# Two expert layers in one program block: the second layer's setup lines up behind the first's last block

## The reference, cut to what matters

```python
# x: 4 sequences x 5056 tokens x 256; N = 20224 tokens, D = 256, E = 8 experts, F = 1024
h[t] = f[t] * h[t-1] + (1 - f[t]) * x[t]          # scan, f from f_logit and lower_bound
# layer 1: every expert takes exactly N/8 tokens, by rank over all (token, expert) logits
y[tokens of e] = relu(h[tokens of e] @ w1[e]) @ w2[e]
# layer 2: every token goes to its best expert, times that expert's softmax weight
e*, g = argmax, softmax of y @ w_gate2
out[t] = g[t] * (relu(y[t] @ w1b[e*]) @ w2b[e*])
```

## Time and profile before

| | us |
|---|---|
| three runs | 2419.19, 2417.88, 2418.66 (median 2418.66) |
| the profiled execution, its own time | 2422.26 |
| its span, from the first to the last instruction | 2420.5 |
| PE busy in the span | 2268.7 (94%) |
| mean granted clock of PE | 0.973 of full |
| last matmul of the first layer's last block, end | 1380.8 |
| first transpose of the second layer, start | 1411.8 |

### The profile page before, as it was taken

How to read it: one execution, slowest core, us unless ns; L and a number is a source line. 1 busy time by engine, 2 the same in 40 slices (tenths; PEclk the granted TensorE clock), 3 DMA queues, 4 the chain that set the end, 5 groups by cost and what they waited for, 6 DMA issues and landing times. The chain is left out here.

```text
span 2420.5 us, 51866 instructions
## 1 busy us (share of the span) xinstructions
PE 2268.7 (94%) x18040; PEld 2114.1 (87%) x18041; DVE 1383.2 (57%) x3375; ACT 810.4 (33%) x2027; POOL 952.2 (39%) x1036
## 2 busy tenths in 40 slices
PE   7883699999999999999999869999999999999997
PEld 7882588888888888888898769999999999999997
DVE  8887876776767677686644433333343333333332
ACT  4440324242332424233333223333333333333332
POOL 5550233333333333333433353535353535335333
PEclk9995699999999999999999979999999999999999
DMA  7894111121211112121221131122121212111111
GB/s 275 289 315 150 53 43 64 42 69 40 71 41 45 66 40 68 42 71 38 77 79 42 43 101 47 42 78 77 43 76 45 78 44 73 47 44 42 41 46 37
DMA packets 86191, 182.95 MB, mean 76 GB/s; under 512 B 14318, under 2 KB 50929, under 8 KB 86066
## 3 DMA queue, kind: packets, MB, share of 16 engines
q0 software_dynamic: 31872, 85.58, 11.4%
q1 hardware_dynamic: 40722, 82.34, 9.7%
q10 hardware_dynamic: 13472, 13.37, 2.0%
HBM read 118.94 MB, written 64.13 MB: 76 GB/s over the span
## 5 line engine op out<-in xcount | busy, mean ns | idle before, releaser
L1853 DVE SCALAR_TENSOR_TENSOR m_hl<-m_hP,m_hh 128x256 fp32r<-128x256 f32 x664 | 274.9, 424 | 531.5 <-ACT m_hh L1812 460.3
L1812 ACT ACTIVATE m_hh<-m_hP 128x256 fp32r<-128x256 f32 x664 | 247.3, 384 | 514.8 <-PE m_hP L1763 510.8
L1085 ACT ACTIVATE m_hh<-m_hP 128x512 fp32r<-128x512 f32 (+1 forms) x320 | 189.8, 593 | 628.2 <-PE m_hP L956 617.0
L824 POOL DMA_INDIRECT y_rows<-spare,m_dest x164 | 182.0, 1110 | 537.4 <-DVE m_dest L1424 488.9
L1384 DVE SCALAR_TENSOR_TENSOR m_hl<-m_hP,m_hh 128x512 fp32r<-128x512 f32 (+1 forms) x320 | 218.5, 683 | 272.0 <-ACT m_hh L1085 253.4
L814 POOL DMA_INDIRECT spare<-h_rows,m_idx x164 | 192.0, 1171 | 56.9 <-issue 37.5
L1701 POOL DMA_INDIRECT m_xg<-y_rows,m_idx x170 | 167.9, 988 | 101.4 <-POOL m_idx L1697 69.5
L1712 POOL DMA_INDIRECT out_dram<-m_rows,m_dest x166 | 168.0, 1012 | 50.6 <-issue 50.6
L1697 POOL COPY m_idx<-rows_i 128x2 int32 (+1 forms) x85 | 15.6, 183 | 409.9 <-ACT m_meta L1816 389.2
L1774 PE MATMUL m_yP<-w_1h,m_hh 128*128 128x256 f32 x672 | 140.7, 291 | 1.3 <-DVE m_hl L1853 1.2
L1774 PE MATMUL m_yP<-w_0h,m_hh 128*128 128x256 f32 x656 | 137.4, 291 | 0.0
(11 more groups left out here) (297 smaller groups left out, 5693.4 us busy)
## 6 DMA issues: line engine op xcount, KB each, us to landing
spare<-in_moe_w_dram SPq DMA_DIRECT2D x32, 1024.0 KB, 6.1
f_in<-in_f_logit_dram SPq DMA_DIRECT2D x39, 512.0 KB, 4.5
x_in<-in_x_dram SPq DMA_DIRECT2D x39, 512.0 KB, 5.3
h_rows<-rows ACTq DMA_DIRECT2D x25, 512.0 KB, 4.5
h_rows<-spare SPq DMA_DIRECT2D x14, 512.0 KB, 6.2
m_xg<-y_rows,m_idx POOLq DMA_INDIRECT x170
out_dram<-m_rows,m_dest POOLq DMA_INDIRECT x166
spare<-h_rows,m_idx POOLq DMA_INDIRECT x164
```

The lines of the kernel that those rows point to most:

```text
L824: pool.indirect_dma_start(dst[:, :], bass.IndirectOffsetOnAxis(ap=dest[:, k:k + 1].bitcast(U32), axis=0), rows[(i - 1) % 2][:, k, 0:ROW].b ...
L1085: act.activation(hh[f % 2][:, tokens(i)], hP[f % 2][:, tokens(i)], ACT.Relu).then_inc(hh_ready, 1)
L1812: act.activation(hh[f % AHEAD][:], hP[f % AHEAD], ACT.Relu).then_inc(hh_ready, 1)
L1853: dve.scalar_tensor_tensor(out=hl[f % AHEAD][:], in0=hP[f % AHEAD], scalar=0.0, in1=hh[f % AHEAD][:].bitcast(F32), op0=ALU.max, op1=ALU.su ...
```

## The change

- `route_and_experts` and `experts_top1` become `first_experts` and `second_experts`. They open no block of their own; each returns its five per-engine functions, and `both_experts` calls, in one block, the first's and then the second's on each engine. The DRAIN and the meeting at L571 are gone; the one at the end stays.
- The second layer has no big tiles of its own. `xg` is the first 2 x 258 columns of the first layer's `rows[0]`, row after row without a gap; `rows` and `meta` lie in its `xg`; `xh`, `xl`, `hh`, `hl` in its `xh[1]`, `xl[1]`, `hh`, `hl`. In PSUM, `hP` is `hP[0]`, `hP[1]`, `yP` 0 and `yP` 1, `yP` is `yP` 2 and 3, and `tP` is `tP` and `bank`: eight banks of one accumulator each, as before.
- The plan on DVE is cut in two. First the block counts, then rows and empty places of blocks 0 to 7 (`plan_rows(0, 8)`), then `c.plan`, then a wait until POOL has issued the last scatter, then `plan_rows(8, 89)`.
- Where the end of the block stood, new waits: POOL waits for its last scatters, the weights' halves, the stored zero row and the rows of blocks 0 to 7 before `gather(0)`, and for the plan and all rows after `gather(1)`; PE and ACT wait for the plan; SP waits until gathers 0 and 1 have landed before it loads any weights of the second layer.

```diff
+FIRST_PLANNED = 8
-def route_and_experts(nc, c, src, w1, w2, w_gate2, w1_next, w2_next, dst):
+def first_experts(nc, c, ctx, src, w1, w2, w_gate2, w1_next, w2_next, dst):
...
         scatter_before(BLOCKS1)
+        pool.sem_inc(scatter_issued, 1)
         pool.wait_ge(gathered, 16 * TPC * (BLOCKS1 + 1))
         pool.wait_ge(scattered, 16 * TPC * (BLOCKS1 + 1))
...
+        def plan_rows(lo, hi):
+            n, here, tiles = hi - lo, slice(lo, hi), slice(lo * T2, hi * T2)
+            ...   # begun, 2 x (part, of_block), held, row_f, row_f, rows_i, skip: as before, on [lo, hi) alone
+        plan_rows(0, FIRST_PLANNED)
+        dve.sem_inc(first_rows_known, 1)
+        st.do(dve.tensor_copy(plan_f[:, 0:E], upto[:]))
+        st.do(dve.tensor_copy(plan_f[:, E:2 * E], start[:]))
+        st.do(dve.tensor_copy(c.plan[:], plan_f[:]))
+        dve.sem_inc(plan_known, 1)
+        dve.wait_ge(scatter_issued, 1)
+        plan_rows(FIRST_PLANNED, NB)
+        dve.sem_inc(all_rows_known, 1)
...
-def experts_top1(nc, c, src, w1, w2, dst):
+def second_experts(nc, c, ctx, one, src, w1, w2, dst):
...
+    xg = flat(one.rows[0])[:, 0:T2 * ROW].rearrange("p (k d) -> p k d", k=T2)
+    rows = flat(one.xg)[:, 0:T2 * D].rearrange("p (k d) -> p k d", k=T2)
+    xh, xl = by_half(one.xh[1]), by_half(one.xl[1])
+    hP = [ap[:, 0:C2] for ap in (one.hP[0], one.hP[1], one.yP[:, 0, :], one.yP[:, 1, :])]
+    yP = [one.yP[:, k, 0:D] for k in range(2, 2 + T2)]
+    tP = [one.tP[:, 0:C2], one.bank[:, 0:C2]]
...
     def on_sp(sp):
+        sp.wait_ge(gathered, 16 * T2 * 2)
         with sp.Fori(1, E) as e:
             sp.wait_ge(split, 4 * e)
             load_weights(sp, c, w1, w2, e, raw)
...
+        pool.wait_ge(one.lows, one.all_splits)
         pool.sem_inc(split, 4)
+        pool.wait_ge(one.zero_stored, 16)
+        pool.wait_ge(one.first_rows_known, 1)
         gather(0, True)
         gather(1)
+        pool.wait_ge(one.plan_known, 1)
+        pool.wait_ge(one.all_rows_known, 1)
         for e in range(E):
...
+def both_experts(nc, c, src, moe_w1, moe_w2, w_gate2, moe2_w1, moe2_w2, between, out):
+    with ExitStack() as ctx:
+        one = first_experts(nc, c, ctx, src, moe_w1, moe_w2, w_gate2, moe2_w1, moe2_w2, between)
+        two = second_experts(nc, c, ctx, one, between, moe2_w1, moe2_w2, out)
+        block = ctx.enter_context(nc.Block())
+        @block.gpsimd
+        def _(pool):
+            one.on_pool(pool)
+            two.on_pool(pool)
+        ...   # and so for sync, tensor, scalar, vector
```

More of the change, by code:

```diff
@@ L570, in route_and_experts @@
     SPLITS = UP_SPLITS + DOWN_SPLITS + 1
-    with ExitStack() as ctx:
[L572 to L729, removed]
-        hits_used = sem("hits_used")
-        rows_known = sem("rows_known")
-        w2_turned = sem("w2_turned")
-        w2_kept = sem("w2_kept")
-        wg_made = sem("wg_made")
-        raw1 = sem("raw1")
-        raw2 = sem("raw2")
-        highs = sem("highs")
-        lows = sem("lows")
-        idx_ready = sem("idx_ready")
-        gathered = sem("gathered")
-        x_turned = sem("x_turned")
-        xh_ready = sem("xh_ready")
-        xl_ready = sem("xl_ready")
-        h_made = sem("h_made")
-        hh_ready = sem("hh_ready")
-        hl_ready = sem("hl_ready")
-        h_used = sem("h_used")
-        rows_ready = sem("rows_ready")
-        lessened = sem("lessened")
-        exps = sem("exps")
-        counts_ready = sem("counts_ready")
-        ranks_made = sem("ranks_made")
-        ranks_read = sem("ranks_read")
-        gate_ready = sem("gate_ready")
-        dest_ready = sem("dest_ready")
-        scattered = sem("scattered")
-        rows_free = sem("rows_free")
-        zero_ready = sem("zero_ready")
-        zero_stored = sem("zero_stored")
-        ready = sem("ready")
-        dv = sem("dv")
-        block = ctx.enter_context(nc.Block())
-        def piece(k, n):
-            b = k % 2
-            if n < UP_SPLITS:
-                at = (slice(None), n // 2, slice(n % 2 * CH, (n % 2 + 1) * CH))
-                raw, parts = c.w1_raw[at], c.w1_s[b]
-            elif n < SPLITS - 1:
-                g = 2 * (n - UP_SPLITS)
-                at = (slice(None), slice(g, g + 2), slice(0, D))
-                raw, parts = c.w2_raw[at], c.w2_s[b]
-            else:
-                at = (slice(None), slice(None), slice(D, D + E))
-                raw, parts = gP[min(k, 1)], c.w2_s[b]
-            return raw, parts[0][at], parts[1][at]
@@ new lines, in first_experts @@
+    place_f = sb("place_f", [P, E, TPC])
+    dest_f = sb("dest_f", [P, TPC])
+    dest = sb("dest", [P, TPC], I32)
+    cnt = sb("cnt", [P, E])
+    blocks = sb("blocks", [P, E])
+    blocks_i = sb("blocks_i", [P, E], I32)
+    upto = sb("upto", [P, E])
+    start = sb("start", [P, E])
+    plan_f = sb("plan_f", [P, 2 * E])
+    shift = sb("shift", [P, 2, E])
+    step = sb("step", [P, 2, E])
+    begun = spare.take(E * (COLS2 // T2)).rearrange("p (e n) -> p e n", e=E)
+    part = spare.take(E * (COLS2 // T2)).rearrange("p (e n) -> p e n", e=E)
@@ L1043, in _ @@
[L1043 to L1052 removed]
+            one.on_pe(pe)
+            two.on_pe(pe)
         @block.scalar
         def _(act):
[L1056 to L1064 removed]
@@ L1883, in hgrn_moe_moe @@
+            one.on_dve(dve)
+            two.on_dve(dve)
 def hgrn_moe_moe(nc, x, f_logit, lower_bound, moe_w_gate, moe_w1, moe_w2, moe2_w_gate, moe2_w1, moe2_w2, out):
```

2126 lines of the change are left out of this document (1161 added, 965 removed).

## The result

Twenty-two runs of each kernel gave 2421.02 us after (2418.17 to 2424.18) and 2416.7 before (2414.78 to 2419.19): a ratio of 1.0018, 95% interval 1.0012 to 1.0024. The change makes the kernel 4.3 us slower; a gain of 4.0 us was forecast. The profiled execution of after took 2419.84 (span 2418.1).

A forecast was written before the change was run, and what follows sets the result against it. PE's matmuls fill 94% of the span, so gains lie only where PE idles, at the layer change: 12.4 - 8.0 - 0.4 = 4.0 us, making 2414.7 from the median 2418.66; range 2409.0 to 2421.0.

The forecast's parts named there:

- The border: Change of layer, from the last scatters to PE's first second-layer work: shorter by 12.4 us, bounds 11.5 to 12.9.
- T: Start of PE's first work of the second layer: forecast at 1399.4, where it was 1411.79.
- The 0.5 for gathers beside the plan: POOL's gather issues at the border, stretched by DVE's wide plan operations beside them: 0.5 us, bounds nothing or 1.4.
- the rival of the colliding plan: Plan's second part on DVE stretches both gather issues by over 1.4; T 2 us later, 2416.7 us; chance 0.15.
- the one of the growing DRAIN: The one DRAIN left, at the end, grows with DMAs to clear: 8.2 us more, 2422.9 us; chance 0.08.
- What is given back: Second layer's first blocks: expert 1's weights come late and delay `hand(0)` and `hand(1)`; 8.0 us, bounds 6.6 to 9.1.
- Only after that does it raise `rows_free`: POOL raises it only after splitting the first half of expert 1's weights, so `hand(0)` runs at +21.7, 6.1 later.
- Past this, POOL has slack: After `hand(1)` POOL idles in each ordinary block, so nothing beyond the 8.0 us is given back.
- The clock at T: PE's half-speed clock after the idle time may return later than before; 0.4 us taken off.
- The aliased tiles and banks cost nothing: Shared tiles and PSUM banks of both layers add no time: banks stay separate, first writers wait for gather 0.
- The forecast for slower, 0.12: Chance that the change makes the kernel measurably slower than before: 0.12.

The follow-up runs named there:

- the second profile of before: The kernel before, unchanged, profiled a second time: span 2416.6, one run of 2418.34 us.
- packed_shifted: Kernel after, with second-layer `xh` and `xl` side by side in `xh[1]` and `xh`, `xl`, `hh`, `hl` moved up 320 bytes: 2413.38 us, 0.9985 of before.
- shifted: Kernel after, with only 320 bytes of padding ahead of `xh`, `xl`, `hh`, `hl`: 2412.73 us, 0.9984 of before.
- pad64: Kernel after, with 64 bytes of padding ahead of `xh`, `xl`, `hh`, `hl`: 2412.66 us, 0.9985 of before.
- the first profile: The profiled execution of the kernel before from which the prediction was made: 2422.26 us, span 2420.5.

## Why the prediction was wrong

**The border** was forecast well. T came 13.1 to 14.0 earlier, counted from the end of PE's work before it, for 12.4 (bounds 11.5 to 12.9); the scatters kept their pace of 1.3, the copy came 1.57 after them for the 1.65 taken, the gather landed in 1.81 for 1.84. The 0.5 for gathers beside the plan wasn't paid: the issues took 1.01 and 0.96, though DVE's operations for the 81 other blocks ran beside them, from 1390.45 to 1397.75. That refutes the rival of the colliding plan, and the DRAIN at the end, 9.22 where it was 9.21, refutes the one of the growing DRAIN.

**"What is given back"** had the right beginning, the wrong path and nearly the right size (8.0, measured 9.5), and the size is luck. The failed sentence is "Only after that does it raise `rows_free`". The raising is an instruction of POOL's queue, which doesn't wait for the arithmetic queued ahead of it: `hand(0)` ran 0.10 us after POOL's first low operation had begun, with 5.0 us of them still to do. So it ran at +17.4, not +21.7, and PE stood for 0.7, not 5.6; `hand(1)` ran at +30.9, not +35.1. The weights themselves were at +15.0 for +14.2: from issue to cast 8.3 us, over my bound of 8.1 and farther from the 6.8 that the page "DMA: Bandwidth & Descriptors" of the Trainium skill would have given as an estimate. Blocks 0 and 1 lost just 2.2 of the 9.5 (against the second profile of before). The other 7.2 came where I expected nothing more: POOL's delay doesn't end in slack. It delays `split`, on which SP's next load waits, and gather 3 behind it. The two were next to each other before as well; 8 us later, the gather's landing is what PE waits for. PE then stood 4.44 and its clock fell. Windows of after, behind that stop:

```profile
1441.70:1442.20 0.50, 0.46 (x5) 0.46 (x5) 0.00 (x0) 0.19 (x1) 0.00 (x0) 1.00 0.01 0
1442.20:1443.20 1.00, 1.00 (x7) 1.00 (x6) 0.58 (x2) 0.65 (x2) 0.18 (x1) 0.57 0.00 0
```

```profile
1443.70:1445.70 2.00, 2.00 (x11) 2.00 (x11) 0.00 (x0) 0.00 (x0) 1.52 (x2) 0.50 0.07 12
1445.70:1455.20 9.50, 9.50 (x82) 9.50 (x80) 3.46 (x8) 3.24 (x9) 2.49 (x3) 1.00 0.16 53
```

It works at 1.2 GHz from about 1442.3 to 1445.7, and block 3 is 1.7 longer than before. "Past this, POOL has slack" was true for each ordinary block and false for the first three, in which it has two experts' weights to split.

**The clock at T**, for whose later return I took 0.4 off, returned at +7.5 (half speed to 1404.8) where it had returned at +5.4. Block 0 was 1.0 longer than in the first profile, and 0.5 longer than in the second, in which it returned at +6.4. This is part of the 9.5.

**"The aliased tiles and banks cost nothing"** is the step that turned the sign. I gave reasons for PSUM banks and for waits, and none for the addresses in SBUF: the up matmuls' pace stood in no term of the sum. The runs show 119.4 ns from start to start in place of 117.0, which cost 7.5 us. With 9.5 given back, but at the old places, the kernel would have gained 4: packed_shifted, shifted and pad64 ran at 2412.7 to 2413.4, 3.8 to 4.6 below the kernel before on the same chip, about as forecast (4.0). The range ended at 2421.0 and the time is 2421.02. The forecast for slower, 0.12, rested on the DRAIN alone. No rival of mine reached into the 79 later blocks, where a nanosecond a matmul is 7.6 us (96 x 79 of them).

**The base** played a part too: the three runs before had a median of 2418.66 and all 22 have 2416.7, so the forecast gain would have ended at 2412.7.

## What to carry to other kernels

When tiles are merged, moved or aliased in a kernel that PE bounds, compare the start-to-start distance of its matmuls before and after, and note the addresses modulo 256 bytes of both operands: 64 bytes of padding were worth 7.5 us here. Measure each layer, since the same shift helped the second and cost the first a little. A new wait on a shared loader has to be followed for as long as the engine behind it has no slack, to the point where the next transfers start; the cheap way out is to send the data earlier, where nothing waits, instead of later. And a semaphore raised by an engine's queue may come before the arithmetic written ahead of it, so a chain must not be priced through it.
